# Slots of the first eight blocks made inside the last block's MLP, and idle matmuls ahead of the experts

## The chip, the core and the metric

The kernel runs on one core of one Trainium2 chip. The metric is the device time of one execution in microseconds (us); the median of three runs is given beside the lowest and the highest. One further execution was profiled, and everything that is said of single instructions comes from it. Engines are called as the profile calls them: PE (TensorE matmuls), PEld (TensorE weight loads), DVE (VectorE), ACT (ScalarE), POOL (GpSimd), SP (the engine that here only issues DMAs).

## What is computed

Three stages follow one another. Everything is float32.

```python
# 1 attention, B=2, H=8, S=576, D=64: only the 32 largest scores of a row are kept
scores = q @ k.T / sqrt(D); kth = 32nd largest of the row
attn = softmax(where(scores >= kth, scores, -1e9)); x = (attn @ v) as 1152 rows of 512
# 2 MLP: 512 -> 2048 -> 512
h = x @ w_in; x = (h * cos(h)) @ w_out
# 3 mixture of 8 experts, each token goes to one, at most 288 tokens to an expert
expert = argmax(x @ w_gate); gate = max softmax probability
pos = number of earlier tokens with the same expert; kept if pos < 288
out[i] = gate[i] * (relu(x[i] @ w1[expert]) @ w2[expert])
```

## The kernel before

The 1152 tokens are nine blocks (`NBLK`) of 128. A loop over blocks does the attention of block i together with the MLP of block i-1 and the end of block i-2, so PE always has matmuls to do. Behind the loop stands a tail written out by hand for the last block, number 8: its MLP, and with it the routing of the tokens to the experts. After that come the eight experts, each taking its rows from a table in DRAM (`slot_rows`). Each engine has its own instruction list, written by hand, and the lists meet only at semaphores; an engine that waits holds back all that stands behind the wait in its list.

In the tail the order of the work is this.

- PE: the down matmuls of block 7, the up matmuls of block 8 (`up_half`, four chunks of 512 hidden values in two halves each), among them the transposes and gate matmuls of block 7, then `ranks(0, last_blk, 0)` behind chunk 2, chunk 3, the down matmuls (`down_half`, four chunks of 12 matmuls of 512 columns), the transposes of the block's result y, its gate matmuls (the logits), `ranks(last_blk, NBLK, 1)`, the two totals, and then `turn_rows`, the transposes of the first expert's rows, which wait for the rows.
- ACT: copies out of PSUM, the cosine by the Sin function (`cosine`, `cosine_chunk`), the rounded high parts of the hidden values (`high_g`, `high_chunk`), then the Exp of the routing of blocks 0 to 7 (`exp_logits`), the high parts of the first expert's first weights (`high_w1`), y, its transpose, its logits and the Exp for block 8.
- DVE: `fraction`, `gated`, `low_g` and the same in chunks for the MLP; the routing. `choose` makes the one-hot choice of the expert, `place` turns it with the ranks out of PE into a slot number for each token. `choose(0, last, 0)` stands early, between the first two `fraction`s; `place(0, last, 0, ...)` stands behind all the MLP work, then `choose` and `place` for block 8, and last `low_w1(0, 0)`, the low parts of the first expert's first weights (four instructions of 128x1024). Each small step is tied to the next by a semaphore (`link`).
- POOL: `send(j, part)` writes the 128 rows of block j to their slots with one indirect DMA each. Blocks 0 to 7 wait for `slot_ready` 1, block 8 for `slot_ready` 2.
- SP: waits for all nine sends, then issues in a row the first expert's rows, its second weights (`w2_raw[0]`), the second expert's rows and both its weights.

The first expert's hidden chunks (`expert`, lines 1259 to 1276) use the PSUM pairs in turn, so chunk 2 waits for `sum_he` of chunk 0 (line 1263). On DVE `sum_he` stands behind two `low_w2`, which wait for ACT's `high_w2`, which waits for the load of `w2_raw[0]`.

Of the kernel before, what the change touches and what calls it, by code (L numbers as in the profile page):

```python
# [8 lines left out]
ALU = mybir.AluOpType  # L9
# [36 lines left out]
LAG = 4  # L46


def build(nc, q_in_d, kt_in, v_in, w_in_d, w_out_d, wg_d, w1_d, w2_d, out):
    y_d = nc.dram_tensor("y_rows", (NBLK - 2, P, DM), F32, kind="Internal").ap()  # L50
    slots_d = nc.dram_tensor("slot_rows", (NSLOT, ROW), F32, kind="Internal").ap()
    with ExitStack() as ctx:
# [6 lines left out]
        def sem(name):  # L59
            return ctx.enter_context(nc.semaphore(name))  # L60
# [80 lines left out]
        def table(*shape):  # L141
# [53 lines left out]
        r_step, r_dif_ready, r_exp_ready, hot_ready, pos_ready, slot_ready = (  # L195
            sem(n) for n in ("r_step", "r_dif_ready", "r_exp_ready", "hot_ready", "pos_ready", "slot_ready"))
# [147 lines left out]
        def _(dve):  # L344
# [91 lines left out]
            def choose(lo, hi, part):  # L436

                wide = [P, hi - lo, NE]
                dve.wait_ge(logits_copied, hi)
                link(nc.vector.tensor_reduce(r_max[:, lo:hi], logits[:, lo:hi, :], AX_X, ALU.max))  # L440
                nc.vector.tensor_tensor(r_dif[:, lo:hi, :], logits[:, lo:hi, :],
                                        r_max[:, lo:hi].unsqueeze(2).broadcast_to(wide),
                                        ALU.subtract).then_inc(r_dif_ready, 1)
                dve.wait_ge(r_dif_ready, part + 1)
                dve.wait_ge(table_step, NTABLES)

                link(nc.vector.tensor_scalar(r_raw[:, lo:hi, :], r_dif[:, lo:hi, :], 0.0, None, ALU.is_ge))
                link(nc.vector.tensor_tensor(r_raw[:, lo:hi, :], r_raw[:, lo:hi, :],
                                             ramp.unsqueeze(1).broadcast_to(wide), ALU.mult))
                link(nc.vector.tensor_reduce(r_max[:, lo:hi], r_raw[:, lo:hi, :], AX_X, ALU.max))  # L450
                ins = nc.vector.tensor_tensor(r_hot[:, lo:hi, :], r_raw[:, lo:hi, :],
                                              r_max[:, lo:hi].unsqueeze(2).broadcast_to(wide), ALU.is_equal)
                if hi < NBLK:

                    for j in range(lo, hi):
                        link(ins)
                        ins = nc.vector.tensor_tensor(seen[:, j + 1, :], seen[:, j, :], r_hot[:, j, :], ALU.add)
                ins.then_inc(hot_ready, 1)
                dve.wait_ge(hot_ready, part + 1)

            def place(lo, hi, part, gate_weight):

                wide = [P, hi - lo, NE]

                dve.wait_ge(r_exp_ready, part + 1)
                link(nc.vector.tensor_reduce(r_sum[:, lo:hi], r_exp[:, lo:hi, :], AX_X, ALU.add))
                link(nc.vector.tensor_scalar(r_sum[:, lo:hi], r_sum[:, lo:hi], 1e-9, None, ALU.add))
                link(nc.vector.reciprocal(gate_weight, r_sum[:, lo:hi]))

                link(nc.vector.tensor_tensor(r_pos[:, lo:hi, :], r_hot[:, lo:hi, :],  # L470
                                             first_slot.unsqueeze(1).broadcast_to(wide), ALU.mult))
                link(nc.vector.tensor_reduce(r_base[:, lo:hi], r_pos[:, lo:hi, :], AX_X, ALU.add))
                dve.wait_ge(pos_ready, part + 1)
                link(nc.vector.tensor_tensor(r_pos[:, lo:hi, :], r_hot[:, lo:hi, :],
                                             p_o[:, NE * lo:NE * hi].rearrange("p (n e) -> p n e", e=NE), ALU.mult))
                link(nc.vector.tensor_reduce(r_rank[:, lo:hi], r_pos[:, lo:hi, :], AX_X, ALU.add))
                link(nc.vector.tensor_tensor(r_base[:, lo:hi], r_base[:, lo:hi], r_rank[:, lo:hi], ALU.add))
                link(nc.vector.tensor_scalar(r_rank[:, lo:hi], r_rank[:, lo:hi], float(CAP), float(NOBODY),
                                             ALU.is_ge, ALU.mult))
                link(nc.vector.tensor_tensor(r_base[:, lo:hi], r_base[:, lo:hi], r_rank[:, lo:hi], ALU.add))  # L480
                nc.vector.tensor_copy(slot[:, lo:hi], r_base[:, lo:hi]).then_inc(slot_ready, 1)
# [16 lines left out]
            choose(0, last, 0)  # L498
            fraction(last, 1, 2 * last + 2, odd_turns_ready)
            gated(last, 0)  # L500
            low_g(last, 0)
# [13 lines left out]
            fraction(last, 2, 2 * last + 3, even_turns_ready)  # L515
            gated_chunk(2)
# [12 lines left out]
            place(0, last, 0, y_all[:, :, DM])  # L529
            choose(last, NBLK, 1)  # L530
            place(last, NBLK, 1, y_now[:, DM:DM + 1])
# [5 lines left out]
            low_w1(0, 0)  # L537
# [63 lines left out]
        def _(pool):  # L601
# [149 lines left out]
        def _(act):  # L751
# [173 lines left out]

            def cosine_chunk(c):
# [16 lines left out]
            def exp_logits(lo, hi, part):  # L943
                act.wait_ge(r_dif_ready, part + 1)
                nc.scalar.activation(r_exp[:, lo:hi, :], r_dif[:, lo:hi, :], ACT.Exp).then_inc(r_exp_ready, 1)

# [8 lines left out]
            exp_logits(0, last, 0)  # L955
# [61 lines left out]
        def _(pe):  # L1017
# [199 lines left out]
            both(up_half, last_blk, 2, own_banks)  # L1217
# [9 lines left out]

            ranks(0, last_blk, 0)
            both(up_half, last_blk, 3, own_banks)
# [8 lines left out]
            mm(totals, ones[:, 0:1], r_hot[:, last_blk, :], start=False, stop=True).then_inc(counted, 1)  # L1238

# [101 lines left out]
```

## Time and profile before

| | us |
|---|---|
| median of 3 runs | 696.5 |
| lowest, highest | 695.64, 697.08 |
| profiled execution, its own time | 699.6 |
| its span from first to last instruction | 697.9 |
| granted clock of TensorE, mean | 0.944 |

| engine | busy us | share |
|---|---|---|
| PE | 631.7 | 91% |
| DVE | 551.5 | 79% |
| ACT | 387.5 | 56% |
| POOL | 379.5 | 54% |

The attention and MLP loop ends near 461 us of the span, the tail of block 8 near 504 us, and the first matmul on an expert's rows starts at 518 us. A row of the timeline gives the start and the length in us, the engine, the line of the kernel, the operation, output and input; in brackets stands how long the engine had been idle and who ended it. The granted clock is 1.00 at 2.4 GHz and 0.50 at 1.2 GHz. The profiled execution took 3.1 us more than the median.

### The profile page before, as it was taken

To read this page: it belongs to the slowest core of one execution; us is meant where nothing else is said; L and a number is where in the kernel's file an instruction comes from. 1 tells how busy PE (TensorE), PEld (TensorE's weight loads), DVE (VectorE), ACT (ScalarE), POOL (GpSimd) and SP (SyncE) were. 2 spreads that over 40 slices of the span, in tenths; PEclk is the share of its full clock that TensorE was granted. 3 is DMA by queue.
4 is the path that set the end of the run, shared out by engine and by line. 5 is a ranking of instruction groups with operands and counts; after the bars stand their busy time and mean duration, and the time that the engine had idled before them with its cause. 6 is when DMAs were issued, how large, how long until landed. Compare 5 with 4: busy or idle time off the path is not lost.

```text
span 697.9 us, 12783 instructions
## 1 busy us (share of the span) xinstructions
PE 631.7 (91%) x4180; PEld 544.3 (78%) x4180; DVE 551.5 (79%) x1009; ACT 387.5 (56%) x603; POOL 379.5 (54%) x278
## 2 busy tenths in 40 slices
PE   4678989999999999999999999989629999999996
PEld 2566977987987887888988979879528888888884
DVE  5999998989899799898899899315526667776673
ACT  2454675485585575675673863734406545556450
POOL 0779896589588688598696795940430111001111
PEclk9955797999999999999999999999859999999999
DMA  8697000000000000000000000050269455676510
GB/s 320 269 364 267 4 9 5 20 5 8 20 8 5 21 8 5 24 5 18 8 4 23 0 0 17 1 193 34 91 215 357 176 185 218 263 282 239 187 36 14
DMA packets 17789, 68.58 MB, mean 98 GB/s; under 512 B 1998, under 2 KB 6606, under 8 KB 15056
## 3 DMA queue, kind: packets, MB, share of 16 engines
q1 hardware_dynamic: 16000, 63.27, 24.0%
q0 software_dynamic: 1744, 4.73, 2.0%
q8 instruction: 26, 0.43, 0.3%
q14 instruction: 19, 0.16, 0.1%
HBM read 54.33 MB, written 14.45 MB: 99 GB/s over the span
## 4 chain that ended last, share of the span: by engine, by line
PE 54%; DVE 15%; issue 11%; POOL 10%; DMA 5%; ACT 4%; DVEq 0%; POOLq 0%; SPq 0%; ACTq 0%
PE p_o L1068 6%; DVE top L360 6%; PE p_a L1105 5%; DVE arena L363 5%; PE p_b L1105 4%; PE p_b L1133 4%; PE p_s L1034 4%; PE p_t L1050 3%; PE p_b L1134 3%; PE p_b L1135 3%; POOL mask L618 3%; POOL arena L622 2%; PE p_o L1288 2%; PE p_o L1290 2%; PE p_o L1289 2%
## 5 line engine op out<-in xcount | busy, mean ns | idle before, releaser
L360 DVE MAX8 top<-arena 128x8 f32<-128x576 f32 x288 | 203.8, 745 | 18.5 <-ACT arena L756 18.3
L363 DVE MATCH_REPLACE8 arena<-top,arena 128x576 f32<-128x576 f32 x216 | 158.5, 740 | 0.0
L618 POOL TENSOR_SCALAR mask<-arena,top 128x576 f32<-128x576 f32 x72 | 129.4, 1797 | 26.4 <-DVE top L360 19.0
L622 POOL TENSOR_TENSOR arena<-arena,mask 128x576 f32<-128x576 f32 x72 | 103.4, 1436 | 26.6 <-ACT arena L770 17.0
L1068 PEld LDWEIGHTS p_o<-arena,probsT 128*128 128x128 f32 x640 | 88.7, 213 | 15.0 <-ACT probsT L777 11.9
L1068 PE MATMUL p_o<-arena,probsT 128*128 128x65 f32 x640 | 90.7, 295 | 8.2 <-ACT probsT L777 8.2
L777 ACT COPY probsT<-p_t 128x640 f32<-128x640 f32 x72 | 50.4, 700 | 64.1 <-PE p_t L1050 63.9
L1050 PE MATMUL p_t<-ident,arena 128*128 128x128 f32 x360 | 59.2, 300 | 18.1 <-POOL arena L622 18.0
L1050 PEld LDWEIGHTS p_t<-ident,arena 128*128 128x128 f32 x360 | 44.8, 155 | 38.5 <-POOL arena L622 27.8
L756 ACT COPY arena<-p_s 128x576 f32<-128x576 f32 x72 | 44.2, 643 | 49.4 <-PE p_s L1034 49.4
L1034 PE MATMUL p_s<-arena,q_sb 64*128 64x224 f32 (+5 forms) x320 | 62.1, 495 | 7.2 <-DMA arena<-in_kt 4.5
L1133 PE MATMUL p_b<-w_out_lo,g_hi 128*128 128x512 f32 x144 | 63.5, 441 | 5.3 <-DVE g_lo L403 5.3
L1105 PE MATMUL p_a<-xT,wff 128*128 128x128 f32 x512 | 63.3, 277 | 0.0
L1105 PE MATMUL p_b<-xT,wff 128*128 128x128 f32 x512 | 63.3, 277 | 0.0
L1105 PEld LDWEIGHTS p_a<-xT,wff 128*128 128x128 f32 x512 | 59.7, 192 | 0.1
L1105 PEld LDWEIGHTS p_b<-xT,wff 128*128 128x128 f32 x512 | 59.7, 192 | 0.1
L734 POOL DMA_INDIRECT out_rows<-turns,wff x8 | 9.6, 1198 | 90.0 <-DVE turns L589 88.2
L1134 PE MATMUL p_b<-w_out_hi,g_hi 128*128 128x512 f32 x144 | 57.9, 402 | 0.0
L1135 PE MATMUL p_b<-w_out_hi,g_lo 128*128 128x512 f32 x144 | 57.8, 402 | 0.0
L1034 PEld LDWEIGHTS p_s<-arena,q_sb 64*128 64x128 f32 (+1 forms) x320 | 39.2, 200 | 19.6 <-issue 13.9
L770 ACT ACTIVATE arena<-arena,nbias 128x576 f32<-128x576 f32 x72 | 53.1, 773 | 0.9
L734 POOL DMA_INDIRECT out_rows<-h_sb,wff x8 | 9.1, 1142 | 74.4 <-DVE h_sb L589 72.6
(162 smaller groups left out, 1274.1 us busy)
## 6 DMA issues: line engine op xcount, KB each, us to landing
arena<-in_w SPq DMA_DIRECT2D x8, 2048.0 KB, 8.8
wff<-in_w SPq DMA_DIRECT2D x8, 2048.0 KB, 9.1
slot_rows<-y_now SPq DMA_DIRECT2D x1, 4626.0 KB, 27.0
wff<-in_w_out SPq DMA_DIRECT2D x1, 4096.0 KB, 20.0
wff<-in_w_in SPq DMA_DIRECT2D x1, 4096.0 KB, 15.1
wff<-slot_rows SPq DMA_DIRECT2D x8, 385.5 KB, 4.0
arena<-in_vones SPq DMA_DIRECT2D x2, 1300.0 KB, 9.5
q_sb<-in_q SPq DMA_DIRECT2D x36, 64.0 KB, 1.9
```

The source lines that it names most:

```text
L360: nc.vector.max(best, src).then_inc(top_step, 1)
L363: nc.vector.match_replace(work[:, a, :], best, src, LOWEST).then_inc(top_step, 1)
L618: nc.gpsimd.tensor_scalar(mask[:], s_sb[:, t, :], top[:, t, TOP_K - 1:TOP_K], None, ALU.is_ge).then_inc(mask_made, 1)
L622: nc.gpsimd.tensor_tensor(probs[:, t % 2, :], probs[:, t % 2, :], mask[:], ALU.mult).then_inc(probs_ready, 1)
L770: nc.scalar.activation(probs[:, t % 2, :], s_sb[:, t, :], ACT.Exp, bias=nbias[:, t:t + 1], scale=SCALE).then_inc(exp_ready, 1)
L1034: last = mm(p_s[q, at + lo:at + hi], q_sb[d, p, q], kT[d, b, p, lo:hi], start=True, stop=True)
L1050: last = nc.tensor.transpose(p_t[:, P * c:P * c + P], probs[:, t % 2, k:k + P], ident[:])
L1068: last = mm(p_o[:, col:col + VC], probsT[:, P * c:P * c + P], vones[batch][:, c, t, :], start=(c == 0), stop=(c == NVC - 1))
L1105: last = mm(bank_c[:, P * n:P * n + P], w_in[:, k, P * f:P * f + P], xT[:, k, :], start=(k == 0), stop=(k == KC - 1))
L1133: mm(p_b[:], g_hi[:, cols], w_out_lo[:, f, :], start=(f == 0), stop=False)
L1134: mm(p_b[:], g_hi[:, cols], w_out_hi[:, f, :], start=False, stop=False)
L1135: last = mm(p_b[:], g_lo[:, cols], w_out_hi[:, f, :], start=False, stop=(f == FC1 - 1))
```

## The change

Five edits, all in the tail.

1. DVE: `place` for blocks 0 to 7 moves up. It is cut into `place_first` (the slot numbers, right behind `gated(last, 0)`) and `weigh_first` (the gate weights, right behind `fraction(last, 2)`), and the sends wait for both through a new semaphore.
2. PE and ACT follow: `ranks(0, last_blk, 0)` moves from behind chunk 2 of the up matmuls to between its halves; the Exp of blocks 0 to 7 moves from behind `high_chunk(3)` to behind `high_g(last, 0)`, that is between two Sin functions.
3. Fewer small DVE instructions: the slot's base comes from the one-hot's maximum by one multiply and add, comparison and multiplication are fused, the slot is written as an integer by the last addition.
4. DVE: `low_w1(0, 0)` stands ahead of the routing of block 8 (`place_last`) and not behind it.
5. PE: behind the totals come 30 matmuls of 512 columns whose result nobody reads (`IDLE_TURNS`).

```diff
-            def place(lo, hi, part, gate_weight):
-                dve.wait_ge(r_exp_ready, part + 1)
...
+            def place_first():
+                at = slice(0, first)
+                link(nc.vector.tensor_scalar(r_base[:, at], r_max[:, at], -float(CAP), float(NE * CAP),
+                                             ALU.mult, ALU.add))
+                dve.wait_ge(pos_ready, 1)
+                link(nc.vector.tensor_tensor(r_pos[:, at, :], r_hot[:, at, :],
+                                             p_o[:, 0:NE * first].rearrange("p (n e) -> p n e", e=NE), ALU.mult))
+                link(nc.vector.tensor_reduce(r_rank[:, at], r_pos[:, at, :], AX_X, ALU.add))
+                link(nc.vector.tensor_tensor(r_base[:, at], r_base[:, at], r_rank[:, at], ALU.add))
+                link(nc.vector.tensor_scalar(r_rank[:, at], r_rank[:, at], float(CAP), float(NOBODY),
                                              ALU.is_ge, ALU.mult))
+                nc.vector.tensor_tensor(slot[:, at], r_base[:, at], r_rank[:, at], ALU.add).then_inc(slot_ready, 1)
+
+            def weigh_first():
+                at = slice(0, first)
+                dve.wait_ge(r_exp_ready, 1)
+                link(nc.vector.tensor_reduce(r_sum[:, at], r_exp[:, at, :], AX_X, ALU.add))
+                link(nc.vector.tensor_scalar(r_sum[:, at], r_sum[:, at], 1e-9, None, ALU.add))
+                nc.vector.reciprocal(y_all[:, :, DM], r_sum[:, at]).then_inc(weight_ready, 1)
+
+            def place_last():
+
+                own = logits[:, first, :]
+                top_own, raw, hot = r_max[:, first:NBLK], r_raw[:, first, :], r_hot[:, first, :]
+                rank, base, total = r_rank[:, first:NBLK], r_base[:, first:NBLK], r_sum[:, first:NBLK]
+                dve.wait_ge(logits_copied, NBLK)
+                link(nc.vector.tensor_reduce(top_own, own, AX_X, ALU.max))
+                nc.vector.tensor_scalar(r_dif[:, first, :], own, top_own, None, ALU.subtract).then_inc(r_dif_ready, 1)
+                link(nc.vector.scalar_tensor_tensor(raw, own, top_own, ramp, ALU.is_ge, ALU.mult))
+                link(nc.vector.tensor_reduce(base, raw, AX_X, ALU.max))
+                nc.vector.tensor_scalar(hot, raw, base, None, ALU.is_equal).then_inc(hot_ready, 1)
+                link(nc.vector.tensor_scalar(base, base, -float(CAP), float(NE * CAP), ALU.mult, ALU.add))
+                dve.wait_ge(r_exp_ready, 2)
+                link(nc.vector.tensor_reduce(total, r_exp[:, first, :], AX_X, ALU.add))
+                link(nc.vector.tensor_scalar(total, total, 1e-9, None, ALU.add))
+                nc.vector.reciprocal(y_now[:, DM:DM + 1], total).then_inc(weight_ready, 1)
+                dve.wait_ge(hot_ready, 2)
+                dve.wait_ge(pos_ready, 2)
+                link(nc.vector.tensor_tensor(r_pos[:, first, :], hot, p_o[:, NE * first:NE * NBLK], ALU.mult))
+                link(nc.vector.tensor_reduce(rank, r_pos[:, first, :], AX_X, ALU.add))
+                link(nc.vector.tensor_scalar(total, rank, float(CAP), float(NOBODY), ALU.is_ge, ALU.mult))
+                nc.vector.tensor_scalar(slot[:, first:NBLK], rank, base, total, ALU.add, ALU.add).then_inc(slot_ready, 1)
...
-            choose(0, last, 0)
+            choose_first()
             fraction(last, 1, 2 * last + 2, odd_turns_ready)
             gated(last, 0)
+            place_first()
             low_g(last, 0)
...
             fraction(last, 2, 2 * last + 3, even_turns_ready)
+            weigh_first()
             gated_chunk(2)
...
-            place(0, last, 0, y_all[:, :, DM])
-            choose(last, NBLK, 1)
-            place(last, NBLK, 1, y_now[:, DM:DM + 1])
+            low_w1(0, 0)
+            place_last()
             dve.wait_ge(counted, 1)
...
-            low_w1(0, 0)
...
                 pool.wait_ge(slot_ready, part + 1)
+                pool.wait_ge(weight_ready, part + 1)
...
             high_g(last, 0)
+            exp_logits(0, last, 0)
...
-            exp_logits(0, last, 0)
             high_w1(0, 0, 0)
...
-            both(up_half, last_blk, 2, own_banks)
+            up_half(last_blk, 2, 0, own_banks)
             ranks(0, last_blk, 0)
+            up_half(last_blk, 2, 1, own_banks)
...
+            for n in range(IDLE_TURNS):
+                mm(p_t[:, 0:512], w_out_hi[:, 0, 0:P], w_out_hi[:, n % FC1, :], start=True, stop=True)
```

## Rows read from the trace of the kernel before

**Rows 1.** Timeline of PE, from the tail into the first expert.

```profile
485.56 0.48 PE L1133 MATMUL p_b<-w_out_lo,g_hi 128*128 128x512 f32 x1
...
518.14 0.87 PE L1248 MATMUL p_a<-ident,wff 96*128 96x96 f32 x4 [15.38 <-DMA wff<-slot_rows]
...
520.81 0.69 PE L1271 MATMUL p_s<-x_parts,w_hi 128*128 128x384 f32 x1 [1.16 <-DVE x_parts L545]
...
521.46 0.58 PE L1271 MATMUL p_s<-x_parts,w_hi 128*128 128x384 f32 x1
...
521.99 0.58 PE L1271 MATMUL p_s<-x_parts,w_hi 128*128 128x384 f32 x1
...
528.35 0.41 PE L1271 MATMUL p_s<-x_parts,w_hi 128*128 128x384 f32 x1 [1.03 <-DVE h_sb L560]
...
533.02 0.49 PE L1248 MATMUL p_a<-ident,wff 96*128 96x96 f32 x4
```

**Rows 2.** The chain that ended last, 496 to 530 us: start, length, what.

```profile
511.02 3.00 DMA slot_rows<-y_now,slot
...
514.46 9.81 DMA arena<-in_w
```

**Rows 3.** POOL's sends: line L722 (ns min/median/max, starts), and the seventh in the timeline.

```profile
L722 POOL DMA_INDIRECT slot_rows<-arena,slot x8: 974/976/4983, 496.6 to 509.7; - x8
...
504.45 4.98 POOL L722 DMA_INDIRECT slot_rows<-arena,slot  x1 [0.30 <-issue]
```

**Rows 4.** Timeline of DVE in the tail.

```profile
484.16 1.23 DVE L403 TENSOR_TENSOR g_lo<-h_sb,g_hi 128x1024 fp32r<-128x1024 f32 x1 [1.11 <-ACT g_hi L807]
...
489.18 0.69 DVE L512 TENSOR_TENSOR g_lo<-h_sb,g_hi 128x512 fp32r<-128x512 f32 x1
...
495.25 0.17 DVE L481 CAST slot<-arena 128x8 int32<-128x8 f32 x1
...
500.34 0.16 DVE L440 TENSOR_REDUCE arena<-logits 128x1 f32<-128x8 f32 x1 [4.91 <-ACT logits L833]
...
502.68 0.16 DVE L474 TENSOR_TENSOR arena<-arena,p_o 128x8 f32<-128x8 f32 x1 [0.20 <-PE p_o L1226]
...
503.65 0.15 DVE L481 CAST slot<-arena 128x1 int32<-128x1 f32 x1
...
503.97 4.61 DVE L526 TENSOR_TENSOR w_lo<-arena,w_hi 128x1024 fp32r<-128x1024 f32 x4
```

**Rows 5.** Timeline of ACT, in the loop (first row) and in the tail.

```profile
454.60 1.28 ACT L802 ACT_TABLE_LOAD   x1 [1.56 <-DVE turns L384]
...
486.48 0.63 ACT L930 ACTIVATE turns<-turns 128x512 f32<-128x512 f32 x1 [2.35 <-DVE turns L384]
...
491.32 1.28 ACT L945 ACT_TABLE_LOAD   x1
492.62 0.26 ACT L945 ACTIVATE arena<-arena 128x64 f32<-128x64 f32 x1
...
497.01 0.59 ACT L825 COPY y_now<-p_b 128x512 f32<-128x512 f32 x1 [0.35 <-PE p_b L1135]
...
500.73 0.21 ACT L945 ACTIVATE arena<-arena 128x8 f32<-128x8 f32 x1 [0.43 <-DVE arena L441]
```

**Rows 6.** Timeline of VectorE and GpSimd in the second expert, 545 to 549 us.

```profile
546.06 2.36 DVE L551 TENSOR_TENSOR w_lo<-wff,w_hi 128x1024 fp32r<-128x1024 f32 x2 [0.45 <-ACT w_hi L978]
...
546.51 1.58 POOL L734 DMA_INDIRECT out_rows<-turns,wff  x1 [0.40 <-issue]
```

**Rows 7.** Timeline of PE early in the loop, behind its one long wait.

```profile
105.38 0.77 PE L1133 MATMUL p_b<-w_out_lo,g_hi 128*128 128x512 f32 x1 [2.96 <-DVE g_lo L403]
```

**Rows 8.** Stretches of PE: length, busy time and matmuls, granted clock, DMA share, GB/s.

```profile
104.00:105.00 1.00, 0.00 (x0) 0.77 0.00 0
...
114.00:115.00 1.00, 1.00 (x5) 0.61 0.00 0
...
524.00:525.00 1.00, 1.00 (x7) 0.81 0.79 277
```

More of the change, by code:

```diff
@@ L46 @@
 LAG = 4
+IDLE_TURNS = 30
 def build(nc, q_in_d, kt_in, v_in, w_in_d, w_out_d, wg_d, w1_d, w2_d, out):
@@ L194, in build @@
         const_step, table_step, nobody_ready, prefilled = sem("const_step"), sem("table_step"), sem("nobody_ready"), sem("prefilled")
-        r_step, r_dif_ready, r_exp_ready, hot_ready, pos_ready, slot_ready = (
-            sem(n) for n in ("r_step", "r_dif_ready", "r_exp_ready", "hot_ready", "pos_ready", "slot_ready"))
+        r_step, r_dif_ready, r_exp_ready, hot_ready, pos_ready, slot_ready, weight_ready = (
+            sem(n) for n in ("r_step", "r_dif_ready", "r_exp_ready", "hot_ready", "pos_ready", "slot_ready",
+                             "weight_ready"))
         rows_sent, last_row_sent = sem("rows_sent"), sem("last_row_sent")
@@ L434, in link @@
                 dve.wait_ge(r_step, steps[0])
[L436 to L442, printed above, removed]
-                                        ALU.subtract).then_inc(r_dif_ready, 1)
[L444 to L457, printed above, removed]
-                ins.then_inc(hot_ready, 1)
-                dve.wait_ge(hot_ready, part + 1)
@@ L461, in place @@
-            def place(lo, hi, part, gate_weight):
-                wide = [P, hi - lo, NE]
-                dve.wait_ge(r_exp_ready, part + 1)
[L466 to L478, printed above, removed]
-                                             ALU.is_ge, ALU.mult))
-                link(nc.vector.tensor_tensor(r_base[:, lo:hi], r_base[:, lo:hi], r_rank[:, lo:hi], ALU.add))
-                nc.vector.tensor_copy(slot[:, lo:hi], r_base[:, lo:hi]).then_inc(slot_ready, 1)
@@ new lines, in _, with choose_first @@
+            first = NBLK - 1
+            def choose_first():
+                wide = [P, first, NE]
+                dve.wait_ge(logits_copied, first)
+                dve.wait_ge(table_step, NTABLES)
+                at = slice(0, first)
+                link(nc.vector.tensor_reduce(r_max[:, at], logits[:, at, :], AX_X, ALU.max))
+                nc.vector.tensor_tensor(r_dif[:, at, :], logits[:, at, :],
+                                        r_max[:, at].unsqueeze(2).broadcast_to(wide),
+                                        ALU.subtract).then_inc(r_dif_ready, 1)
+                dve.wait_ge(r_dif_ready, 1)
+                link(nc.vector.scalar_tensor_tensor(r_raw[:, at, :], r_dif[:, at, :], 0.0,
+                                                    ramp.unsqueeze(1).broadcast_to(wide), ALU.is_ge, ALU.mult))
+                link(nc.vector.tensor_reduce(r_max[:, at], r_raw[:, at, :], AX_X, ALU.max))
+                ins = nc.vector.tensor_tensor(r_hot[:, at, :], r_raw[:, at, :],
+                                              r_max[:, at].unsqueeze(2).broadcast_to(wide), ALU.is_equal)
+                for j in range(first):
+                    link(ins)
+                    ins = nc.vector.tensor_tensor(seen[:, j + 1, :], seen[:, j, :], r_hot[:, j, :], ALU.add)
+                ins.then_inc(hot_ready, 1)
+                dve.wait_ge(hot_ready, 1)
@@ new lines, in weigh_first @@
+            def weigh_first():
+                at = slice(0, first)
+                dve.wait_ge(r_exp_ready, 1)
[23 more added lines that the diff above has]
+                nc.vector.tensor_scalar(slot[:, first:NBLK], rank, base, total, ALU.add, ALU.add).then_inc(slot_ready, 1)
@@ L924, in _, with exp_logits @@
             high_g(last, 0)
+            def exp_logits(lo, hi, part):
+                act.wait_ge(r_dif_ready, part + 1)
+                nc.scalar.activation(r_exp[:, lo:hi, :], r_dif[:, lo:hi, :], ACT.Exp).then_inc(r_exp_ready, 1)
+            exp_logits(0, last, 0)
             def cosine_chunk(c):
@@ L941, in _ @@
             high_chunk(3)
-            def exp_logits(lo, hi, part):
-                act.wait_ge(r_dif_ready, part + 1)
-                nc.scalar.activation(r_exp[:, lo:hi, :], r_dif[:, lo:hi, :], ACT.Exp).then_inc(r_exp_ready, 1)
             def high_w1(E, j, turn):
```

## Prediction

> **What bounds the kernel now.** I read PE's timeline first, since PE is busy 91% of the span and any long hole in it is worth asking about. There is one: the transposes of the first expert's rows start at 518.14 us after 15.38 us in which PE waits for the DMA of the rows, and behind them chunk 0 of the expert starts at 520.81. A second, short hole (1.03 us) ends at 528.35, where chunk 2 starts [rows 1]. The chain of waits says what fills both: the last send (`slot_rows<-y_now`) starts at 511.02 and takes 3.00 us to land, then SP issues the loads, and the second weights land 9.81 us after their issue at 514.46 [rows 2]; ACT rounds them, DVE makes two low parts and then `sum_he`, and that releases chunk 2 at 528.35. So up to 528.35 everything hangs on when the last send starts, and from then on PE is busy without a break.
>
> Why does the last send start at 511.02? The rows of the sends: they begin at 496.6, because the slots of blocks 0 to 7 are made behind the MLP, and the seventh, at 504.45, takes 4.98 us where the median is 0.98 [rows 3]. DVE's timeline gives the reason: at 503.97 the four `low_w1` instructions begin and run 4.61 us, to 508.58, and the slow send ends 0.85 us after them, at 509.43 [rows 3, 4]. The slot of block 8 itself was ready at 503.65 + 0.15 = 503.80 [rows 4]. From there to 511.02 are 7.2 us in which only POOL is late.
>
> **Edit 1, the eight sends in the MLP.** `place_first` is six small steps at about 0.2 us, 1.3 us. It lies in the 1.11 us in which DVE waits for ACT's `g_hi` ahead of 484.16 [rows 4]; what sticks out is 0.2 us. `ranks` one half chunk earlier puts its four matmuls before `h_ready` of chunk 2, so ACT's copy and `g_hi` also end a little later (some 0.2, by a first guess): the same 0.2, not a second one. The gate weights are ready after `fraction(2)` plus 0.65 us, near 487.4. A send starts 1.0 us after its release (496.6 against the slots' end at 495.42) [rows 3, 4], so the sends run from about 488.5. At 0.98 us and 0.30 of issue each [rows 3], eight take 10.2 us. If they got nowhere at all during the four `low_w1` (about 493.8 to 498.4 in the new order), four are done before and four behind, by 503.6. If every DVE instruction in 488.5 to 493.8 held them too, so that only two were done by 493.8, the eighth ends at 506.1. The last send's slot comes at 504.0 and it could start at 505.0 (below), so the queue costs 0 to 1.1 us. I take 0: the slow send [rows 3] was held by four instructions without a gap, and between the MLP's DVE instructions there are gaps.
>
> Rather than being held, could the sends hold DVE? In the second expert a send begins at 546.51, inside two `low_w2` of DVE that begin at 546.06 and take 2.36 us together, 1.18 each, against 4.61 / 4 = 1.15 of the same shape [rows 4]; the send takes 1.58 us instead of about 1 [rows 6]. So POOL waits for DVE and DVE doesn't wait for POOL. The Trainium skill says otherwise (page SBUF — State Buffer, section "Who interferes with whom"): an instruction of DVE with two inputs in SBUF and one of POOL that reads SBUF exclude each other, and whichever starts first keeps the other out to its end. In its first direction the trace agrees (4.98 us), in the second it doesn't; by the rule the MLP would be held as the third rival says.
>
> **Edit 2, the Exp between two Sins.** A table load takes 1.28 us and stands behind the wait of the instruction that needs it: in the loop it began only when DVE had released the Sin, after 1.56 us of idling [rows 5]. Before, the tail had one load for Exp, at 491.32, off the path. Now there are three: Exp at about 484.4 (free: ACT idled 2.35 us there [rows 5]), Sin again, which begins when `fraction(2)` is ready at 486.7 (0.2 late), and Exp again for block 8. The second makes the Sin of chunk 2 start at 486.7 + 1.28 + 0.02 = 488.0 where it started at 486.48, 1.5 us later. `low_chunk(2)` ends 1.5 us later too, at 489.18 + 0.69 + 1.55 = 491.4 [rows 4]. PE wants it behind 24 down matmuls: 48 of them took from 485.56 to 497.01, 0.238 us each, so it was wanted at 491.2 [rows 1, 5]. PE is about 0.4 us late with the down matmuls, the 0.15 us of the later start included. Chunk 3 is ready at 493.6 and wanted at 494.3: no cost. Between 0.15 (the load comes ahead of its wait) and 0.8 us, I take 0.4. By the figure of the Trainium skill for a change of table set (page ScalarE: Activation LUTs, section "What ACT_TABLE_LOAD costs": 1.28 us for the load, as in the row, and 1.38 more for a drain) the path would be 1.4 us later here and 1.4 later below; the rows show the Exp at 492.62, 1.30 us behind the start of its load at 491.32 and so with no drain, and they decide [rows 5].
>
> **Edit 3, `place_last`.** Counted from DVE's first instruction on the logits at 500.34 [rows 4]: the difference is out at 500.70, ACT takes it at 500.73 [rows 5]; now 1.28 us of table load come ahead of the Exp of 0.21, so it ends at 502.25. Three DVE steps of 0.2 (five took 502.68 to 503.65 [rows 4]) give the weight at 502.85. The ranks were read at 502.68 [rows 4], they come 0.2 earlier now and are no longer last. Four steps more, 0.8 us, end at 503.6, against 503.80. Two effects cancel: the shorter chain gains about a microsecond and the table load takes most of it back. With the 0.4 of edit 2 the slot is ready at 504.0.
>
> **Edit 4, `low_w1` ahead.** 4.61 us of DVE work [rows 4] go into its idle time between 493.6 and 500.7 (behind `high_w1` on ACT, about 492.8 to 496.7). Behind `place_last` DVE has nothing of weight, so nothing holds the last send: it starts at 504.0 + 1.0 = 505.0, with 0.1 either way. Sum of edits 1 to 4: 511.02 - 505.0 = **6.0 us** earlier. Landing, loads and rounding behind it keep their lengths, since SP issues the same transfers in the same order; the rows reach PE at 512.1 and chunk 2 can start at 522.35.
>
> **Edit 5, the idle matmuls.** They start behind the totals at about 503. At 2.4 GHz a matmul of 512 columns takes 0.238, thirty take 7.1 us; at 1.2 GHz twice that, an estimate of 14.3. The clock had stood at half for the whole hole and came back at 524.4, 3.6 us after chunk 0 began [rows 1, 8]. With the same 3.6 us at half (about 7.5 matmuls) and the rest full they end at 503 + 3.6 + 5.4 = 512.0, as the rows arrive. So chunks 0 and 1 likely run at full clock: chunks 2 and 3 took 533.02 - 528.35 = 4.7 us [rows 1], against 528.35 - 1.03 - 520.81 = 6.5 for chunks 0 and 1 (1.03 is the hole ahead of chunk 2). What is that worth? Nothing: chunk 2 waits for the second weights, at 522.35 however fast chunk 1 was.
>
> And it opens a new hole. Chunk 0 starts at 512.1 + 2.2 = 514.3 (it was 2.67 behind the rows, with the transposes at half clock; 2.2 is my estimate at full), chunk 1 ends at 519.0, and PE stands still for **3.4 us** until 522.35, where before it was 1.0. In the loop a wait of 2.96 us was enough: the clock went to half during it and came back only near 114.6, 9.2 us after work resumed [rows 7, 8]. So chunks 2 and 3 likely start at 1.2 GHz, now on the path. A pair of matmuls takes 521.99 - 521.46 = 0.53 at half clock [rows 1] and 4.67 / 16 = 0.29 at full. For 3.6 us at half, work worth 3.6 x 0.29 / 0.53 = 1.95 is done: **1.65 us lost**. For 9.2 us it is 4.2. The loss lies between 0 (the clock holds) and 4.2; I take 1.65, since chunks 2 and 3 are the same kind of matmuls as the ones that took 3.6.
>
> **The sum.** 699.6 (the profiled execution's own time, of which 697.9 are span) - 6.0 + 1.65 = 695.2, which is 4.35 less. The runs' median is 3.1 under that execution, so 696.5 - 4.35 = **692.1**. With the loss at 4.2 it is 694.7; with 3 us of half clock, 691.9.
>
> **The rivals.**
> - The clock holds. The hole may be too short, or lie so that the clock stays, or chunks 0 and 1 run partly at half and fill it (the transposes and the 1.2 us wait behind them are thin work). Then all of the 6.0 stays: 690.5. Against it: the 2.96 us wait [rows 7]. Chance 0.27.
> - The sends are starved: each waits for DVE in the MLP, and only two are through at 498.4. Six take 7.7 us, the last starts at 506.1 to 506.5: gain 6.0 - 1.3 - 1.65 = 3.0, 693.5. With none through at 498.4 it starts at 508.6, 695.7. For it: the 4.98 us. Against: the 1.58 us send shows one passing between two back-to-back instructions [rows 6]. Chance 0.09.
> - The sends hold DVE, each up to 0.98 us, at five instructions on the MLP's path from 488.6 to 493.5: chunk 3 up to 4.9 us later, less its 0.7 of slack, PE 4.2 later and the gain 6.0 - 4.2 - 1.65 = 0.2: 696.3, no change. Against: [rows 6]. Chance 0.04. (The rule of the Trainium skill, page SBUF — State Buffer, names this case.)
> - Slower: the idle matmuls don't bring the clock back and only block PE. Thirty at half clock end at 503 + 14.3 = 517.3, the transposes and their wait take 2.7, and the chunks 0 to 3 take 4 x 8 x 0.53 = 17.0 us: chunk 3 ends at 537.0 where it ended at 533.02: 4.0 slower, 700.5. It turns from gain to loss when chunk 3 ends later than 533.02. For it: 9.2 us at half clock under steady work once [rows 7, 8], and a hole of 15 us that left it at half. Chance 0.04.
> - The change doesn't do what it says: the eight sends begin late for a reason outside my rows (a semaphore that comes with the y load, POOL's own list), and the last one starts where it did: 696.5 to 696, within 0.2%. Chance 0.04.
> - The forecast, the clock lost for a time behind the new hole: 0.52.
>
> **How the numbers follow.** The range goes from the held clock with 0.7 us of luck in the latencies, 689.8, to the long loss of clock with a little of the send queue, 695.0. Outside lie the last three rivals and the tails, under 0.2. A measurement of this kernel can tell about 0.2%, 1.4 us, from no change: below 695.1 is faster. Faster 0.88 (forecast, held clock and most of the starved sends), same 0.07, slower 0.05.
>
> **What the profile after would show.** POOL: eight sends from 488.5, most near 0.98 us, one or two longer across `low_w1`; the last from 505.0. DVE: no instruction of the MLP longer than before. ACT: three table loads from 484 on. PE: down matmuls ending 0.4 us later, thirty matmuls of 512 columns from 503 to about 512, the granted clock up within them, a hole near 3.4 us ahead of chunk 2, and a clock of 0.50 behind it for 3 to 4 us. The prediction is wrong if the last send starts later than 506, if PE's hole ahead of chunk 2 is under 2 us, or if the clock stays at 1.00 across it.

## The result: 7 us faster, more than forecast

| | before | changed |
|---|---|---|
| median, 16 runs each | 696.56 us | 690.13 us |
| lowest, highest | 692.33, 700.53 | 683.47, 693.63 |
| profiled execution, its span | 697.9 | 686.6 |

The ratio of changed to before is 0.9896, with a 95% interval of 0.9877 to 0.9914: 7.2 us faster, 6.0 to 8.6. The forecast was 4.35 us, 692.1. The median lies in the range as a number, but the ratio taken on the 696.5 of the forecast gives 689.3, half a microsecond under its lower end. The direction was right and the size was too small. One run of an experiment below (b_w1_ahead) took 1200.91 us and is left out of its ratio.

The two profiled spans are 11.3 us apart, and not all of that is the change. At the start of the tail, the copy of the block's x on ACT (`xT<-p_a`), the changed kernel is already 3.39 us ahead (463.46 against 460.07), in code that the change doesn't touch. These two rows, of the stretches of PE (length, busy time and matmuls, granted clock, DMA share, GB/s), show one difference, the granted clock; the first is of the kernel before, the second of the changed one.

```profile
0.00:60.00 60.00, 39.52 (x158) 0.80 0.87 326
```

```profile
0.00:60.00 60.00, 40.64 (x163) 0.99 0.87 327
```

They don't explain the lead alone: a second profile of the changed kernel (a_same2 below) has 0.99 there too and reaches the same copy at 462.57. Its clock from 60 to 120 us is 0.78, against 0.77 before and 0.84 in the changed kernel. Over the fourteen profiles of this document the copy starts anywhere from 459.14 to 463.46, so whole spans carry up to 4.3 us from ahead of the tail. So I measure in the tail: from the start of ACT's copy of y (`y_now<-p_b`) to the last send, and on to PE's transposes behind chunk 3 of the first expert. Timeline of the changed kernel, POOL first, then ACT, SP and PE; start, length, engine, line, operation, and in brackets the idle time ahead of it and who ended it.

```profile
484.96 1.23 POOL L745 DMA_INDIRECT slot_rows<-arena,slot  x1 [26.43 <-issue]
486.49 0.98 POOL L745 DMA_INDIRECT slot_rows<-arena,slot  x1 [0.30 <-issue]
...
490.49 1.18 POOL L745 DMA_INDIRECT slot_rows<-arena,slot  x1 [0.30 <-issue]
491.97 1.97 POOL L745 DMA_INDIRECT slot_rows<-arena,slot  x1 [0.30 <-issue]
...
495.52 0.97 POOL L745 DMA_INDIRECT slot_rows<-arena,slot  x1 [0.30 <-issue]
500.77 0.97 POOL L745 DMA_INDIRECT slot_rows<-y_now,slot  x1 [4.28 <-DVE slot L503]
```

```profile
493.74 0.58 ACT L848 COPY y_now<-p_b 128x512 f32<-128x512 f32 x1 [1.33 <-PE p_b L1159]
...
504.10 0.44 SPq L330 DMA_DIRECT2D arena<-in_w  x1
...
512.50 2.00 ACT L1002 CAST w_hi<-arena 128x1024 fp32r<-128x1024 f32 x2 [3.60 <-DMA arena<-in_w]
```

```profile
498.86 8.70 PE L1267 MATMUL p_t<-w_out_hi 128*128 128x512 f32 x30
507.48 0.52 PE L1277 MATMUL p_a<-ident,wff 96*128 96x96 f32 x4
...
509.63 0.45 PE L1300 MATMUL p_s<-x_parts,w_hi 128*128 128x384 f32 x1 [1.29 <-DVE x_parts L567]
516.56 0.66 PE L1300 MATMUL p_s<-x_parts,w_hi 128*128 128x384 f32 x1 [2.07 <-DVE h_sb L582]
522.77 0.49 PE L1277 MATMUL p_a<-ident,wff 96*128 96x96 f32 x4
```

The eight sends are done at 496.49. The last slot is ready at 499.97, 3.5 us later, so POOL now waits for DVE, where before the last send followed the eighth after 0.30 us of issue. The last send starts 7.03 us behind the copy of y and not 14.01. The idle matmuls end at the rows. The hole ahead of chunk 2 is there, 2.07 us where it was 1.03 [rows 1], and chunks 2 and 3 take 522.77 - 516.56 = 6.21 us where they took 4.67. From the copy of y to the transposes behind chunk 3 it is 29.03 us; before it was 533.02 - 497.01 = 36.01 [rows 1, 5].

### The profile page after: what moved, and what is told of

Same layout as the page of the kernel before. It is cut to its first block, busy times and chain, and to the rows that moved or that the text cites. A ratio compares the mean times of both kernels' runs of the same rounds, so it can differ in the third digit from the quotient of the medians.

```text
span 686.6 us, 12837 instructions
## 1 busy us (share of the span) xinstructions
PE 636.3 (93%) x4210; PEld 547.5 (80%) x4210; DVE 550.3 (80%) x1002; ACT 389.9 (57%) x605; POOL 375.8 (55%) x278
## 4 chain that ended last, share of the span: by engine, by line
PE 61%; DVE 14%; issue 9%; POOL 6%; ACT 5%; DMA 3%; DVEq 1%; POOLq 0%; ACTq 0%; SPq 0%
PE p_o L1092 8%; PE p_a L1129 5%; DVE top L362 5%; PE p_s L1058 4%; DVE arena L365 4%; PE p_t L1074 4%; PE p_b L1129 4%; PE p_b L1157 3%; PE p_b L1159 3%; PE p_b L1158 3%; PE p_s L1300 2%; DVE g_lo L405 2%; PE p_t L1300 2%; PE p_o L1317 2%; PE p_o L1319 2%
```

## The experiments

The table has one profile of each kernel. "Last send" is its start and "chunk 3 done" the start of PE's transposes behind it, both from the start of the copy of y; "load" goes from the issue of the first expert's second weights to ACT's first use of them ("half" where the load is cut in two and ACT begins on the first half); "hole" is PE's idle time ahead of chunk 2. A dash means that there was no hole to part chunk 1 from chunk 2. The changed kernel was profiled three times. The ratios are to runs of the kernel before on the same chip, with the 95% interval. All times in us.

| kernel | last send | load | hole | chunks 2 and 3 | chunk 3 done | ratio |
|---|---|---|---|---|---|---|
| before | 14.01 | 9.83 | 1.03 | 4.67 | 36.01 | 1 |
| changed | 7.03 | 8.40 | 2.07 | 6.21 | 29.03 | 0.9896 (0.9877 to 0.9914) |
| changed, a_same2 | 7.19 | 8.68 | 1.82 | 6.25 | 29.54 | 0.9920 (0.9896 to 0.9943) |
| changed, a_same3 | 7.03 | 8.81 | 2.24 | 4.68 | 28.19 | 0.9894 (0.9864 to 0.9924) |
| a_w1_behind | 7.04 | 10.75 | 0.54 | 4.66 | 33.77 | 0.9951 (0.9931 to 0.9971) |
| b_w1_ahead | 11.78 | 9.30 | none | - | 33.17 | 0.9983 (0.9959 to 1.0007) |
| a_exp_behind | 9.23 | 9.42 | 0.43 | 4.67 | 30.81 | 0.9928 (0.9903 to 0.9952) |
| a_preload | 7.19 | 8.87 | 1.98 | 6.24 | 29.80 | 0.9890 (0.9866 to 0.9914) |
| a_no_idle | 7.03 | 9.66 | none | - | 28.82 | 0.9898 (0.9869 to 0.9927) |
| a_fill | 7.18 | 8.65 | filled | - | 28.08 | 0.9891 (0.9846 to 0.9935) |
| a_w2_alone | 7.34 | 9.83 | 2.58 | 4.68 | 29.33 | 0.9880 (0.9834 to 0.9926) |
| a_split | 7.19 | 5.61, half | none | - | 26.07 | 0.9867 (0.9835 to 0.9899) |
| a_split2, the same | 7.04 | 6.00, half | none | - | 25.63 | 0.9840 (0.9789 to 0.9890) |
| a_split_no_idle | 7.04 | 5.88, half | none | - | 28.77 | 0.9896 (0.9833 to 0.9960) |

**Does VectorE hold GpSimd's sends?** (a_w1_behind)

```diff
-            low_w1(0, 0)
             place_last()
...
+            low_w1(0, 0)
```

> The changed kernel with low_w1 back behind the last block's slots and second_round. Theory (VectorE's four 128x1024 subtractions keep GpSimd's send from its work): the send of block 8, released at the same time, takes near 4.9 us and not 0.98, ends about 0.9 us behind the last subtraction, and the kernel is 3.5 to 4.5 us slower than the changed one. Rival (the slow seventh send of the kernel before was a matter of the queue of sends, of its ring or its writes): the ninth send takes about 1 us, nothing is lost.

Measured: the send took 4.83 us. DVE's and POOL's rows of this kernel's timeline:

```profile
501.67 4.61 DVE L550 TENSOR_TENSOR w_lo<-arena,w_hi 128x1024 fp32r<-128x1024 f32 x4
```

```profile
502.31 4.83 POOL L745 DMA_INDIRECT slot_rows<-y_now,slot  x1 [5.48 <-DVE slot L503]
```

It is a single send behind an idle queue, so a full ring of sends can't be the cause. It ends 0.86 us behind the last subtraction, as the seventh send of before did (0.85). Against the changed kernel's first ratio the kernel loses about 3.8 us of the 7.2 (0.0055 of 696.5), as expected. The first theory holds.

**Is the order of low_w1 enough by itself?** (b_w1_ahead, made from the kernel before)

```diff
             place(0, last, 0, y_all[:, :, DM])
+            low_w1(0, 0)
             choose(last, NBLK, 1)
...
-            low_w1(0, 0)
```

> The kernel before with edit 4 alone: low_w1 stands behind the slots of blocks 0 to 7 and ahead of the last block's routing. Theory (the sends need VectorE to leave them alone and need 10.2 us for eight; both must move): the first send is held until low_w1 ends (about 3.5 us more), no send is held later, eight end near 509.5 in the frame of the kernel before, the last send starts 0.5 to 1.5 us earlier than before, the kernel gains 1 us or less. Rival (the one slow send was the whole cost): it gains 4 us.

The last send starts 2.2 us earlier, more than the 0.5 to 1.5 expected, and the whole gains 1.2 us, with an interval that reaches no change. The sends began inside `low_w1` and were held far less than in the experiment before:

```profile
494.96 2.18 POOL L722 DMA_INDIRECT slot_rows<-arena,slot  x1 [34.65 <-issue]
497.45 1.77 POOL L722 DMA_INDIRECT slot_rows<-arena,slot  x1 [0.30 <-issue]
499.52 0.97 POOL L722 DMA_INDIRECT slot_rows<-arena,slot  x1 [0.30 <-issue]
...
507.20 0.97 POOL L722 DMA_INDIRECT slot_rows<-y_now,slot  x1 [0.30 <-issue]
```

But the last slot was ready at 502.84 (DVE, line 481) and its send went at 507.20: the eight others stood ahead of it. So neither edit 4 alone nor, as a_w1_behind shows, the early sends with a late `low_w1` bring the 7 us; it takes both. The rival's 4 us are out as well.

**What do the early gate weights do?** (a_exp_behind: the Exp of blocks 0 to 7 and `weigh_first` back behind the MLP)

```diff
             high_g(last, 0)
-            exp_logits(0, last, 0)
...
+            exp_logits(0, last, 0)
             high_w1(0, 0, 0)
...
-            weigh_first()
             gated_chunk(2)
...
+            weigh_first()
             low_w1(0, 0)
```

> The changed kernel with the Exp of blocks 0 to 7 and their gate weights back behind the MLP, the slots still early. Theory (what lets the eight sends start early is the weights, and what they need is 10.2 us of GpSimd that low_w1 doesn't hold): the sends start near 7 us later than in the changed kernel, inside low_w1, the first two take about 2 us each, the last send starts 2.5 to 4 us later against the copy of y, and the kernel is 2.5 to 4 us slower than the changed one. The Sin of chunk 2 needs no table load and comes 0.5 us earlier, which PE doesn't notice. Rival (the sends only need to be done before the last block's slot comes, whatever their start): no difference.

The sends start 6.5 us later and back to back up to the last, which starts 2.2 us later than in the changed kernel, at 504.60, though its slot was ready at 501.34. The loss is 1.8 us in the medians of one chip (692.14 against 690.37), under the 2.5 to 4 expected, because again two sends inside `low_w1` took 1.39 and 1.77 us and no more. The direction is right. This kernel also has no table load between the two Sins, and its y is copied 33.67 us behind xT, as in the changed kernel (493.74 - 460.07).

**Does the table load cost anything?** (a_preload)

```diff
             cosine_chunk(3)
+            nc.scalar.activation(nbias[:], nbias[:], ACT.Exp)
             high_chunk(3)
```

> The changed kernel with one more Exp on a tile that nobody reads, right behind the last Sin, so that the table for Exp is in place when the last block's logits come. Theory (the table load of 1.28 us stands between the logits and the Exp, and VectorE waits 0.5 us for it): no table load behind the logits, the last send starts 0.3 to 0.6 us earlier against the copy of y, the kernel is 0.3 to 0.6 us faster, less than three rounds can tell. Rival (the extra load delays the last low part of the MLP, and PE with it): y is copied later against the start of the tail, the gain is given back.

There is no load behind the logits any more, and PE is not late (y is copied 33.68 us behind xT, 33.67 in the changed kernel). Yet the last send starts at 7.19 us, since DVE waits for the ranks instead. The first row is PE's first two matmuls of `ranks`, the second is DVE's:

```profile
497.43 0.59 PE L1249 MATMUL p_o<-arena 128*128 128x8 f32 x2 [1.31 <-DVE arena L492]
```

```profile
498.56 0.16 DVE L500 TENSOR_TENSOR arena<-arena,p_o 128x8 f32<-128x8 f32 x1 [0.54 <-PE p_o L1250]
```

But these ranks ran at a granted clock of 0.50, where the profile of the changed kernel had them at 1.00 and in 0.39 us. The profile to compare it with is a_same2, whose ranks ran at 0.50 too: 7.19 us as well, with the load. So at half clock the load costs nothing, and for full clock this profile can't tell. Another kernel can: in a_exp_behind the table for Exp was in place as well, and its ranks ran at full clock. Rows of ACT, PE and DVE:

```profile
499.20 0.21 ACT L951 ACTIVATE arena<-arena 128x8 f32<-128x8 f32 x1 [0.54 <-DVE arena L489]
```

```profile
499.77 0.39 PE L1247 MATMUL p_o<-arena 128*128 128x8 f32 x2 [1.31 <-DVE arena L492]
```

```profile
501.07 0.27 DVE L503 TENSOR_SCALAR slot<-arena 128x1 int32<-128x1 f32 x1
```

From the copy of y, at 495.37, to its slot it is 5.97 us, against 6.23 in the changed kernel. So at full clock the load behind the logits costs 0.26 us.

**What are the idle matmuls worth here?** (a_no_idle: `IDLE_TURNS = 0`)

> The changed kernel without its 30 idle matmuls. Theory 1 (they bring the clock back for chunks 0 and 1 of the first expert, but chunk 2 waits for the second weights all the same, and the longer hole ahead of it costs clock): chunks 0 and 1 take 6.5 us at half clock, the hole ahead of chunk 2 shrinks from 2.07 us to under 1 us, chunks 2 and 3 take 4.7 us and not 6.2, so the kernel is 0.5 to 1.5 us faster than the changed one (about 8 us faster than before). Rival (a cold start of the expert reaches past the landing of the weights and costs more than the hole): 1 to 2 us slower than the changed kernel, chunk 2 starts later against the last send than the 15.8 us of the changed kernel.

The same time as the changed kernel: 0.9898 against 0.9896, and 28.82 us to the end of chunk 3 against 28.19 to 29.54. The interval of the ratio is 2 us wide on either side, so it doesn't exclude the 0.5 us expected at least. The hole is gone and with it the fall of the clock, as expected. Two things eat the gain, and they end together. The load of the second weights takes 9.66 us, about 1 us more than with the idle matmuls, and releases chunk 2 near 519.5 (4.06 us behind ACT's first use at 515.48, as in the changed kernel). But PE is busy until then too: chunks 0 and 1 took 519.53 - 511.93 = 7.60 us and not 6.5, since the clock came back only 6.1 us behind the start of chunk 0, where it took 3.6 before. A shorter load would have gained 0.1 us at most (chunk 1's last matmul at 519.24 and the usual 0.20 behind it). PE's stretches and the start of chunk 2:

```profile
517.00:518.00 1.00, 1.00 (x6) 0.50 0.92 393
518.00:519.00 1.00, 1.00 (x8) 0.98 1.19 508
```

```profile
519.53 0.41 PE L1300 MATMUL p_s<-x_parts,w_hi 128*128 128x384 f32 x1
```

**Is it the hole that costs the clock?** (a_fill)

```diff
                     wait(pe, w1_lo_made, 4 * E + c + 1)
+                    if isinstance(E, int) and E == 0 and c == 2:
+                        for f in range(9):
+                            mm(p_o[:, 0:512], w_out_hi[:, 0, 0:P], w_out_hi[:, f, :], start=True, stop=True)
```

> The changed kernel with nine more idle matmuls of 512 columns (2.1 us) ahead of chunk 2 of the first expert, where PE stands still for 2.07 us. Theory (that hole costs the clock): the clock stays at 1.00, chunks 2 and 3 take 4.7 us where they took 6.2, the kernel is 1.5 us faster than the changed one. Rival (the clock falls for another reason, as the thin transposes ahead of chunk 0): chunks 2 and 3 take 6.2 us again, no gain, or 0.5 us lost where the nine reach past the release.

The clock stayed at 1.00, and chunk 3 is done at 28.08 us, 0.95 to 1.5 less than in the two profiles of the changed kernel whose clock fell and 0.1 less than in the one whose clock held. In the ratio, 0.9891 with an interval of 0.0045 either way, that can't be told. The profile agrees with the first theory, but doesn't decide it: the clock also held once in the changed kernel as it is (a_same3, below).

**The changed kernel twice more.**

> The changed kernel once more, unchanged, for a second profile of the same instructions. If the fall of the clock in the hole ahead of chunk 2 is sure, the clock is 0.50 behind it again and chunks 2 and 3 take 6.2 us; if it is a matter of how the hole lies in time, they may take 4.7 us. The second weights' load takes somewhere from 8.4 to 10 us, with no part of the program changed.

> The changed kernel a third time, on the same chip as the three others of this group. The clock falls in the hole ahead of chunk 2 or doesn't, with 1.5 us between the two for chunks 2 and 3; the last send starts 7.0 to 7.3 us behind the start of the copy of y, whatever the clock does.

In a_same2 the clock fell, in a_same3 it held, with the longer hole. Stretches of PE (length, busy time and matmuls, granted clock, DMA share, GB/s), a_same2 first:

```profile
518.00:519.00 1.00, 0.00 (x0) 1.00 0.89 377
519.00:520.00 1.00, 0.46 (x3) 0.90 1.15 492
520.00:521.00 1.00, 1.00 (x5) 0.50 0.97 410
```

```profile
518.00:519.00 1.00, 0.00 (x0) 1.00 1.08 459
519.00:520.00 1.00, 0.66 (x5) 1.00 0.88 377
520.00:521.00 1.00, 1.00 (x9) 1.00 1.09 459
```

Over all profiles with a hole of this size the clock fell behind 1.82, 1.98 and 2.07 us and held across 2.24 and 2.58. It isn't the length alone, and it costs 1.55 us where it happens.

**Is the load slowed by those behind it?** (a_w2_alone)

```diff
             expert_rows(1, 1, 0)
+            sp.wait_ge(w2_in[0], 16)
```

> The changed kernel, but SP waits for the landing of the first expert's second weights before it issues the second expert's weights (4 MB). Theory (the 8.4 to 9.8 us of that load are shared with 4 MB behind it): it lands in 5 to 6.5 us, chunk 2 starts 2 us earlier or more, PE's hole ahead of it closes, the clock holds, and the kernel is 2 to 3.5 us faster than the changed one. Rival (the load goes through its queue in order and the others behind it cost it nothing; what varies is the chip): it takes 8.4 us again, no gain, and the second expert's weights come 3 us later with no harm.

The load took 9.83 us with nothing but two small row loads beside it. That is more than the 8.4 of the rival, and its direction is right: what is issued behind the load isn't what makes it long. The second expert's weights were issued some 9 us later, with no loss that shows. The ratio, 0.9880, doesn't differ from that of the changed kernel by more than its interval.

**Is the load the bound?** (a_split, a_split2)

```diff
-            sp.dma_start(w2_raw[0], w2_d[0]).then_inc(w2_in[0], 16)
+            sp.dma_start(w2_raw[0][:, 0:FC2 // 2, :], w2_d[0][:, 0:FC2 // 2, :]).then_inc(w2_half_in, 16)
+            sp.dma_start(w2_raw[0][:, FC2 // 2:FC2, :], w2_d[0][:, FC2 // 2:FC2, :]).then_inc(w2_in[0], 16)
...
-                if c == 0:
+                if c == (2 if isinstance(E, int) and E == 0 else 0):
                     wait(act, w2_in[j], 16 * (turn + 1))
+                if c == 0:
                     if isinstance(E, int) and E == 0:
+                        act.wait_ge(w2_half_in, 16)
```

> The changed kernel with the load of the first expert's second weights cut in two halves with a semaphore each, so that ACT can round the first half while the second is on its way. Theory (chunk 2 of the first expert waits for nothing but that load, and the idle matmuls have already made chunks 0 and 1 fast): the first half lands 4 to 5 us earlier, chunk 2 starts as soon as chunk 1 ends, 2 us earlier, the clock has no hole to fall in, and the kernel is 2 to 3.5 us faster than the changed one. Rival (the halves land together, because the load's pieces are spread over the same queues): no gain.

> The split kernel once more, on the chip of the kernel without idle matmuls. It should be 2 to 3.5 us faster than the changed kernel again, with PE busy from chunk 0 on and the clock at 1.00 through chunks 2 and 3.

Rows of a_split: ACT begins on the first half as it comes, and PE has no hole from chunk 0 to the transposes behind chunk 3.

```profile
509.11 2.00 ACT L1005 CAST w_hi<-arena 128x1024 fp32r<-128x1024 f32 x2 [0.21 <-DMA arena<-in_w]
```

```profile
509.63 0.44 PE L1303 MATMUL p_s<-x_parts,w_hi 128*128 128x384 f32 x1 [1.29 <-DVE x_parts L568]
518.92 0.49 PE L1280 MATMUL p_a<-ident,wff 96*128 96x96 f32 x4
```

Chunks 0 to 3 take 9.3 us, twice the 4.67 of two chunks at full clock. ACT begins 5.61 and 6.00 us behind the issue, some 3 us earlier than in the changed kernel and not 4 to 5, which was enough. Against the changed kernel on the same chip the medians are 4.7 and 3.6 us lower (686.51 and 691.21; 686.81 and 690.37). That is more than the 2 to 3.5 expected; the profiles (26.07 and 25.63 us against 28.19 to 29.54) say 3.1 on the mean. Against before the kernel is at 0.9867 and 0.9840, some 9 to 11 us; it beats both.

**And the idle matmuls there?** (a_split_no_idle: both edits)

> The changed kernel with the split load of the second weights and without the idle matmuls. Theory (the idle matmuls are worth something only where nothing else is late): chunks 0 and 1 at half clock end 2 us later than in the split kernel, nothing waits between them and chunk 2, and the kernel is 1.5 to 2.5 us slower than the split kernel with its idle matmuls. Rival (the idle matmuls are worth nothing anywhere): the same time.

3.1 us slower than a_split2 in the medians of one chip (689.92 against 686.81), 28.77 against 25.63 us in the profiles. PE runs the first 5.7 us of chunks 0 and 1 at half clock, with no wait ahead of chunk 2:

```profile
511.30 0.69 PE L1303 MATMUL p_s<-x_parts,w_hi 128*128 128x384 f32 x1 [1.16 <-DVE x_parts L568]
523.21 0.50 PE L1280 MATMUL p_a<-ident,wff 96*128 96x96 f32 x4
```

More than the 1.5 to 2.5 expected. The interval of this ratio alone is wide (0.9833 to 0.9960), so the amount rests on the two profiles: 11.91 us for the four chunks against 9.30.

## Why the forecast was too low

The mechanism held: the last send came free of the queue and of `low_w1`, and a hole with a fall of the clock opened ahead of chunk 2. What failed are three sizes in the sum: the load of the second weights (kept at 9.83 us, it took 8.63 on the mean), the length of the slot's path (6.0 us, it was 6.86), and the loss by the clock (1.65 us taken whole, it came in two of three profiles).

**The sends (edits 1 and 4).** Right in mechanism. The eight sends ended long before the last slot, and the last send found POOL free. Across `low_w1` one took 1.18 and one 1.97 us, where the forecast had reckoned that none might get through. The sends didn't hold DVE: its instructions of the MLP that ran beside them took 0.69 us as before, one of them 0.74 [rows 4]. So the second direction of the rule of the Trainium skill (page SBUF — State Buffer, section "Who interferes with whom", the first to start keeps the other out) isn't seen here, and its rival is out; the first direction is, at 4.83 us.

**The length of the slot's path (edits 2 and 3): mis-sized, on a wrong premise.** I had 6.0 us for the start of the last send; from the copy of xT it is 33.67 + 7.03 = 40.70 against 33.55 + 14.01 = 47.56, so 6.86. The premise that a table load stands behind the wait of its instruction, read from one row of the loop [rows 5], is wrong for the tail:

```profile
482.21 0.26 ACT L951 ACTIVATE arena<-arena 128x64 f32<-128x64 f32 x1
482.49 1.28 ACT L959 ACT_TABLE_LOAD   x1
483.78 0.63 ACT L959 ACTIVATE turns<-turns 128x512 f32<-128x512 f32 x1
...
496.87 0.17 ACT L856 COPY logits<-p_a 128x8 f32<-128x8 f32 x1 [1.21 <-PE p_a L1185]
497.05 1.28 ACT L951 ACT_TABLE_LOAD   x1
498.34 0.21 ACT L951 ACTIVATE arena<-arena 128x8 f32<-128x8 f32 x1
```

The Sin's load starts right behind the Exp, 0.7 us before DVE's `fraction` is ready (483.22); the last one starts at 497.05, 0.4 us before the difference that the Exp reads is ready (497.49). So both run in part while ACT would have waited. Why the load in the loop stood behind its wait wasn't tried. In the code the Sin there waits for two semaphores (`cosine`), these two for one each; that fits, and is no more than a guess. PE was late by 0.12 us and not 0.4, and a_exp_behind, without a load between the Sins, was late by the same 0.12: the load cost PE nothing. The path from y to the slot fell by 0.56 us (6.79 to 6.23; in a_same2, where the last ranks ran at half clock, to 6.39) and not 0.2. The difference of 0.36 is the premise's: the Exp ends 1.49 us behind DVE's first step and not 1.91. The remaining 0.2 is the start of the send, 0.80 us behind its slot and not 1.0. Edit 3 was never run by itself, so how much of the 0.56 its fewer steps are worth is not shown. There is no drain behind a load (Exp 1.29 us behind the load's start), so on this the row keeps deciding against the figure of the Trainium skill (page ScalarE: Activation LUTs, section "What ACT_TABLE_LOAD costs").

**The load of the second weights: a term that I held constant.** I kept its 9.83 us. It took 8.40, 8.68 and 8.81 us in the three profiles of the changed kernel, 8.63 on the mean, which is 1.2 us that the sum didn't have and its largest error. The cause stays open: nothing that the change does to DMA explains it, and all that the profiles show is the correlation told at the end.

**The clock behind the new hole: right in size, but taken whole.** Forecast 1.65 us lost, with a chance of 0.27 that nothing is; measured 6.23 - 4.68 = 1.55, in two of three profiles, so about 1.0 on the mean. The hole was forecast at 3.4 us and was 1.8 to 2.2, since the load was shorter. The row that I took for proof, a clock that fell during 2.96 us [rows 7], doesn't carry over: 2.24 and 2.58 us were survived, 1.82 wasn't. What else decides stays open. (Its length was also misread a little: a granted clock of 0.61 in 114 to 115 means half clock up to about 114.8, not 114.6.) Two of the three profiles show one of the signs that I had named for a wrong prediction: a hole under 2 us in a_same2, a clock that stays at 1.00 in a_same3.

**The sum again, with measured terms:** 6.86 + 1.2 - 1.0 = 7.1 us, against 7.2 measured. The forecast was 6.0 - 1.65 = 4.35. Of the 2.8 us between, 0.9 is the slot's path and the send's start, 1.2 the load, 0.65 the clock. With the first two put right the sum gives 690.05, still inside the range; it takes the third as well to fall below 689.8. My range was too narrow below because it had only 0.7 us for shorter latencies, and none for a load that differs.

**Edit 5** was forecast to be worth nothing in time, and as it stands the runs show no worth (a_no_idle). What it gives (full clock in chunks 0 and 1) goes into a wait; a_split2 and a_split_no_idle show that it is worth 3 us as soon as that wait is gone.

## What to carry to other kernels

A queue of small indirect sends needs the time of its engine, so start it as soon as its data is there and keep long subtractions of VectorE away from the one send that everything waits for; here `low_w1` ahead brought 1.2 us without the early sends, the early sends 3.4 without `low_w1` ahead, and both 7.2. Before warming an engine's clock, look what the warmed work waits for next: the idle matmuls were worth nothing that the runs could tell until the load behind them was cut in two. And a price read from one profile of a DMA may not hold in the next kernel: here the same load took 8.40 to 10.75 us, so give it a range. Before you say what ate a gain, look whether the engine that waits was free at all (in a_no_idle it wasn't), and whether the granted clock was the same in both profiles (in a_preload it wasn't).

## What the hardware showed beyond that

- Four VectorE subtractions whose inputs were all ready kept a send out to their end (4.83 us and 4.98 us). Where ACT was still making the inputs when they began, as in the changed kernel, b_w1_ahead and a_exp_behind, sends passed between them at 1.2 to 2.2 us each. That what counts is whether the subtractions already stand in the queue fits these rows, but wasn't tried by itself.
- Where chunk 0 began at a granted clock of 0.50, the clock came back to 1.00 after 3.3 us in a_exp_behind, 3.6 in before and 6.1 in a_no_idle, under the same matmuls. So the half-clock time of one profile isn't a price for the next kernel either.
- The load of 2 MB took 8.40 to 8.87 us in the five profiles in which PE was at full clock when the rows came and the loads were issued in the same order, and 9.30 to 10.75 us in the five in which it was at half clock (before, b_w1_ahead, a_exp_behind, a_w1_behind, a_no_idle). Two of the slow ones had the idle matmuls, too early to help. I have no mechanism for it; it is a correlation over ten profiles, and a_w2_alone, with another order of issue, took 9.83 at full clock.
